# VectorE's program for twenty expert groups, written out in place of a loop over experts

## The reference, cut to what matters

```python
p_packed = sm_attn(p, k, v)                  # 32 packed queries per head
x = sm_attn(q, p_packed, p_packed)           # attention over the 32 packed rows, 4 x 8 heads, 576 tokens
x = x.transpose(0, 2, 1, 3).reshape(2304, 512)
logits = x @ w_gate                          # 8 experts
P = exp(logits - logits.max())
for _ in range(8):                           # rows and columns scaled in turn
    P /= P.sum(1, keepdims=True) + 1e-09
    P /= P.sum(0, keepdims=True) + 1e-09
    P *= N / E
for e in range(8):                           # every token goes through every expert
    out += P[:, e:e+1] * (np.maximum(x @ w1[e], 0.0) @ w2[e])     # 512 -> 1024 -> 512
h = out @ w_in                               # 512 -> 2048
return (s * np.maximum(h, 0)**2 + b) @ w_out # 2048 -> 512
```

## Time and profile before

| | |
|---|---|
| median of 3 runs | 1733.7 us (1733.49 to 1736.25) |
| profiled execution, own time | 1731.23 us |
| its span | 1729.4 us |
| mean granted TensorE clock | 0.997 of full speed |
| PE busy | 1707.5 us, 99% |
| DVE busy | 1195.0 us, 69% |
| POOL busy | 1030.3 us, 60% |
| ACT busy | 736.4 us, 43% |

### The profile page before, as it was taken

One profiled execution on the slowest core, in us unless ns is written; L12 is line 12 of the kernel. 1 busy time (PEld: TensorE's weight loads), 2 busy tenths in 40 slices (PEclk: granted clock), 3 DMA queues, 4 the chain that ended last, 5 costly groups with the idle time before them and its releaser, 6 DMA issues.

```text
span 1729.4 us, 30251 instructions
## 1 busy us (share of the span) xinstructions
PE 1707.5 (99%) x9933; PEld 1479.4 (86%) x9933; DVE 1195.0 (69%) x2119; ACT 736.4 (43%) x1672; POOL 1030.3 (60%) x1200
## 2 busy tenths in 40 slices
PE   9999999999999999999999999999999999999999
PEld 7888888888888888888888888888888888888887
DVE  4846646778787778777867867787887555555545
ACT  5644466455454444444444544544533222222222
POOL 1266669888888788788878887788873011111100
PEclk9999999999999999999999999999999999999999
DMA  9431111111112111111112111111101000000002
GB/s 277 120 82 40 47 37 25 38 49 37 37 46 52 37 37 37 49 37 37 37 37 61 37 37 37 49 37 37 48 27 37 13 13 25 25 25 24 0 0 109
DMA packets 71807, 79.09 MB, mean 46 GB/s; under 512 B 7984, under 2 KB 59184, under 8 KB 71728
## 3 DMA queue, kind: packets, MB, share of 16 engines
q1 hardware_dynamic: 71728, 78.15, 16.8%
HBM read 73.42 MB, written 4.72 MB: 45 GB/s over the span
## 4 chain that ended last, share of the span: by engine, by line
PE 94%; POOL 2%; issue 1%; ACT 1%; DMA 1%; DVE 0%; SPq 0%; DVEq 0%; POOLq 0%; ACTq 0%
PE PS L1497 92%; PE PS L1517 2%; ACT g_raw L786 1%; DMA stage<-moe_w_dram 0%; PE PS L1731 0%; POOL w_lo L610 0%; DMA k_raw<-k_dram 0%; POOL span_late L699 0%; POOL w_hi L608 0%; POOL recombined L683 0%; POOL sums_of_a L691 0%; POOL w_lo L625 0%; DVE snaps L1375 0%; POOL span_late L701 0%; POOL a_parts L703 0%
## 5 line engine op out<-in xcount | busy, mean ns | idle before, releaser
L1497 PE MATMUL PS<-w_hi,h_hi 128*128 128x512 f32 x1440 | 566.0, 393 | 0.6 <-DVE acc L1239 0.6
L1497 PE MATMUL PS<-w_lo,h_hi 128*128 128x512 f32 x1440 | 564.5, 392 | 0.0
L1497 PE MATMUL PS<-w_hi,h_lo 128*128 128x512 f32 x1440 | 561.9, 390 | 0.0
L1239 DVE SCALAR_TENSOR_TENSOR acc<-PS,gate,acc 128x512 f32<-128x512 f32 x504 | 378.2, 751 | 186.5 <-PE PS L1497 186.5
L786 ACT ACTIVATE g_raw<-PS 32x256 f32<-32x256 f32 x992 | 372.6, 376 | 16.7 <-PE PS L1497 4.7
L1497 PEld LDWEIGHTS PS<-w_hi,h_lo 128*128 128x128 f32 x1440 | 271.3, 188 | 58.6
L1497 PEld LDWEIGHTS PS<-w_hi,h_hi 128*128 128x128 f32 x1440 | 271.6, 189 | 51.1 <-DVE acc L1239 0.8
L1497 PEld LDWEIGHTS PS<-w_lo,h_hi 128*128 128x128 f32 x1440 | 271.7, 189 | 46.8
L1002 ACT ACTIVATE h_hi<-PS 128x576 fp32r<-128x576 f32 x216 | 129.0, 650 | 317.2 <-DVE PS L1375 317.2
L1497 PE MATMUL PS<-a_parts,g_slots 128*128 128x288 f32 x1296 | 225.8, 296 | 13.5 <-DVE snaps L1375 13.3
L608 POOL CAST w_hi<-stage 128x1024 fp32r<-128x1024 f32 (+1 forms) x78 | 76.7, 983 | 248.1 <-PE PS L1497 217.7
(11 more groups left out here) (158 smaller groups left out, 2161.2 us busy)
## 6 DMA issues: line engine op xcount, KB each, us to landing
stage<-moe_w_dram SPq DMA_DIRECT2D x96, 512.0 KB, 4.9
k_raw<-k_dram SPq DMA_DIRECT2D x8, 512.0 KB, 6.3
q_raw<-q_dram SPq DMA_DIRECT2D x8, 512.0 KB, 5.7
v_raw<-v_dram SPq DMA_DIRECT2D x8, 512.0 KB, 6.5
stage<-moe_w_in_dram SPq DMA_DIRECT2D x16, 256.0 KB, 2.8
stage<-moe_w_out_dram SPq DMA_DIRECT2D x8, 512.0 KB, 3.5
out_dram<-acc SPq DMA_DIRECT2D x16, 256.0 KB, 2.2
p_twice<-p_dram SPq DMA_DIRECT2D x8, 64.0 KB, 4.7
```

What stands on the lines that cost most here:

```text
L1239: return nc.vector.scalar_tensor_tensor(out=dst, in0=y, scalar=share, in1=dst, op0=ALU.mult, op1=ALU.add)
L1497: return nc.tensor.matmul(dst, lhsT, rhs, start=start, stop=stop)
```

## The change

The loop over experts on VectorE, and the three written-out groups behind it, become one Python loop that writes out groups 8 to 30. The expert's column of `gate` is then a constant address, where it was an address from a register. No other engine's program changes, and no piece of arithmetic.

```diff
             def shared(e):
                 def add(dst, y, tile):
-                    share = gate[:, tile, ds(e, 1)]
+                    share = gate[:, tile, e:e + 1]
                     return nc.vector.scalar_tensor_tensor(out=dst, in0=y, scalar=share, in1=dst,
...
             for n in range(1, PER_EXPERT):
                 group_of_seven(UNSCALED + n, shared(1))
-            with dve.Fori(2, E - 1) as e:
-                for n in range(PER_EXPERT):
-                    group_of_seven(e * PER_EXPERT + n, shared(e))
-            for n in range(PER_EXPERT - 1):
-                group_of_seven(MOE_GROUPS - PER_EXPERT + n, shared(E - 1))
+            for g in range(SEVEN + PER_EXPERT - 1, MOE_GROUPS - 1):
+                group_of_seven(g, shared(g // PER_EXPERT))
```

## The result

| | before | after |
|---|---|---|
| median | 1733.6 us (4 runs, 1730.98 to 1736.25) | 1713.67 us (4 runs, 1711.41 to 1718.63) |
| ratio | | 0.9889, 95% interval 0.986 to 0.9918 |
| profiled execution, own time | 1731.23 us | 1715.88 us |
| its span | 1729.4 us | 1714.1 us |

Faster by 1.1%, at 1713.67 us where 1714.3 us was forecast. First the page of the kernel after: busy time, granted clock in 40 slices, and the instruction queue.

A forecast was written before the change was run, and what follows sets the result against it. TensorE, busy 99%, was taken as the bound, standing only behind VectorE's four jumps back. Idle time 13.3, clock 5.0 and restarts 1.1 us made 19.4 us, so 1733.7 - 19.4 = 1714.3 us, range 1710.9 to 1721.0 us.

The forecast's parts named there:

- The jump back, and nothing else at that place: VectorE's four 4.0 us pauses at turn ends of the expert loop belong to fetching instructions at the jump's target.
- Price 19.4 us: Four jumps back in the expert groups cost the end 19.4 us, 4.85 each, measured by distances of last tiles.
- The third term: TensorE's restarts behind the four pauses: 1.1 us, a quarter us each, put to the filling of an empty pipeline.
- The size of the clock's term: Lower TensorE clock behind three of four pauses loses 5.0 us; total gain 15.4 to 21.1 us depending on falls.
- Nothing comes late next: Behind the removed jumps no other wait takes over; groups keep TensorE's own pace of 37.7 us, cost 0.
- Rival A: Only TensorE's idle time at the four pauses comes back, 13.3 us, giving 1720.4 us; 5%.
- Rival C: GpSimd's blocks or ScalarE's tiles come late at the four places, halving the gain: 1724.0 us; 4%.
- Rival D: The last layer's shifted VectorE loop pauses at its two jumps back, taking back 9.7 us: 1724.0 us; 5%.
- Rival B: The pause belongs to the change of expert, not the jump, so nothing changes: 1733.7 us; 3%.
- No price for more code: VectorE's longer straight code in the expert groups is fetched ahead without pauses; cost taken as 0.
- rival E: Straight code in groups 8 to 27 waits for its fetch at 11 packet ends, 4.85 us each: 1767.7 us; 3%.
- The profile after: Expected signs: no VectorE issue idle or TensorE snaps waits, clock 1.00 from group 5, PE busy some 5 us less.

The follow-up runs named there:

- e3: Against the kernel before: VectorE's loop kept for experts 2 to 4 (two jumps back), experts 5 and 6 written out; 1723.99 us.
- e1: Against the kernel before: five VectorE loops of one group a turn (115 instructions, 15 jumps back) in place of one of four groups; 1711.71 us.
- e4: Against the kernel before: VectorE loop of three groups a turn (356 instructions, 5 jumps back), groups 26 and 27 written out; 1711.27 us.
- e5: Against the kernel before: loop of three groups a turn (356 instructions), with 20 already satisfied waits of VectorE added ahead of it; 1738.01 us.
- e11: Against the kernel before: SyncE's first weight loads of groups 14, 18, 22 and 26 delayed, so none run during VectorE's four jumps back; 1718.91 us.
- e8: Against the kernel after: one unused VectorE reduction, an estimated 4 us, added ahead of the joins at four group boundaries, no jump back; 1734.93 us.
- e7: Against the kernel before: four-group loop turned by one piece, so the four jumps back stand behind the joins of a turn's first unit; 1718.74 us.
- e6: Against the kernel after: VectorE's loop of the last layer (134 instructions, two jumps back) written out too; 1711.86 us.
- e9: The kernel after repeated without an edit, for a second trace; 1711.72 us, ratio interval to the kernel before 0.9817 to 0.9898.
- e10: Against the kernel before: four-group loop turned by one unit, so jumps back come some 14 us later, where no weights come in; 1729.36 us.

## Why the prediction was right

**The jump back, and nothing else at that place.** Right, and now shown from three sides: pauses follow the jumps (e3), not the experts; fifteen and five jumps back with shorter bodies are free (e1, e4); the same body in another place pauses (e5). One reading was loose: the packet does not come at the start of the pause but 2.1 to 2.3 us into it, and e11 shows why that matters.

**Price 19.4 us.** The stretch gave back 18.9 us, and the 0.5 us between is a cost of the written-out code (below). The idle time, 13.3 us, is gone whole, and e8 shows that the clock's share is a consequence of it. The third term, 1.1 us at four restarts, is borne out in size. It stands alone in e7 and e11, whose clock never fell: their stretches are 5.4 and 8.8 us over e1's 791.84, TensorE stood 3.9 and 7.1 us, and 1.5 and 1.7 us are left, some 0.4 a pause. The six products behind the pause at 718 us take 1.16 us in the earlier trace rows at a clock of 1.00, and six such products in an ordinary unit 0.96 to 0.97. Its name, "the filling of an empty pipeline", is not shown: e8, without jump and register instructions, leaves only some 0.7 us, and no run separates TensorE's restart from slower joins behind a jump. (The 18.0 us of gain for falls behind two pauses would be 18.2 by its own prices of 5.28 and 3.84 us, which changes nothing.)

**The size of the clock's term.** I took it from one execution, 5 us, and gave up to 21.1 us of gain if the clock fell behind all four pauses. That bound was too low. Timed executions of the kernel before on another chip had a mean clock of 0.988 to 0.998 and took 1745.1 to 1729.17 us, 1736.51 us in the median; the written-out one had 0.999 to 1.0 and took 1711.3 to 1713.09 us. There the gain was 24.8 us. 1% of clock is 17 us, so most of that spread is clock, and e8 shows a fall that costs nearly twice as much as those of the earlier trace rows.

**The median is closer than the working.** 1714.3 us holds 2.5 us by which the timed runs of the kernel before lay above the profiled one, as something that the change does not touch. The repeat does not bear this out: its median is 1711.72 us, which is 1731.2 - 19.4 = 1711.8 without the 2.5. The first four executions after lie in two pairs, 1711.41 and 1711.46 us at a clock of 1.00, and 1715.88 and 1718.63 at 0.999 and 0.997; for 1715.88 the trace has the fall in the attention, for 1718.63 there is no trace. 1713.67 us is the middle between the pairs. So the mechanism and the 19.4 us were right, and that the median came within 0.7 us is luck in part.

**Nothing comes late next.** Right: in the written-out part TensorE's matmuls wait for nobody in the view of waits, and all groups but two are 37.71 us apart. Rival A is out, since more than its 13.3 us came back and the clock stayed at 1.00. Rival C is out. Rival D is out by e6. Rival B is out by e3.

**No price for more code.** Nearly right. The stretch of e1, with its loops, is 0.52 us shorter than that of the written-out kernel. In all four traces of written-out groups (after, e6, e8, e9), groups 11 and 19 are each 0.24 to 0.28 us longer than 37.71. The first of the two places in the kernel after, TensorE's weight load:

```profile
544.33 0.43 PEld L1494 LDWEIGHTS PS<-a_parts,g_slots 128*128 128x128 f32 x3 [0.23 <-DVE snaps L1375]
```

VectorE's joins start at 542.88 and 543.82 us there, 0.94 us apart where it is 0.5 to 0.6 elsewhere; a packet of q14 starts at 544.48, and the same stands at 837.49 us with a packet at 837.65. TensorE's standstills behind VectorE at these two places, with no others in the stretch, are the 0.5 us. The reading is that the crossing into the next piece of the program holds back a join: rival E then exists at 0.26 us in place of 4.85, at two of eleven packets. It rests on the coincidence with the packets, and no run moved them. Eleven packets came in the stretch of 21 groups, 67 to 75 us apart, ten of them in the twenty groups for which eleven, one in some 69 us, had been estimated.

**The profile after.** No issue entry, no wait of the matmuls on `snaps`, clock at 1.00 in the groups, 5.0 us less busy time of TensorE: all as forecast, but for the two weight loads above and a fall of the clock in the attention.

## What to carry to other kernels

VectorE's loops cost nothing here as long as the jump's target was still held (bodies of 115, 134 and, in one place, 356 instructions); look for idle time with "issue" as its end that returns with the loop's period, and shrink the body (one group a turn did as well as writing out all twenty, with some 740 instructions less) or write it out. Price a standstill of TensorE by the distance of equal points of the work and not by the idle time alone, since the clock can fall behind it, and take that part from several executions. A fetch of instructions shares the DMA engines with the kernel's own loads (4.4 us beside them, 3.1 without), so an unavoidable jump belongs where none run and where the waiting engine has work in hand, as in e11 and e7.

## What the runs showed of the hardware that I had not expected

Fetching the program at a jump took 4.3 to 4.8 us beside a weights' load (before, e3, e5), 2.75 to 3.1 us without one in e7 and e11, and 3.5 to 3.8 us without one in e10. The Trainium skill, "Runtime: NRT & Kernel Launch", section "Instruction fetch mechanics", has the fetch from the engine's own DMA queue and a held window of two blocks of 16 KiB; the traces agree on the queue and show packets of 8 KB on q14 (30 of them are 0.25 MB), and four of them, in place of two blocks, have to be held to explain e4 and e5.

Standstills of 3.3 us were followed by a granted clock of 1.00 or 0.72 over 6 us in the kernel before, and of 0.72 or 0.50 in e8, in different places of the same program. In e8 the clock was already at 0.50 while TensorE still stood. A standstill of 0.9 to 2.0 us (e7, e11) was followed by no fall in eight cases.
